# Three of a kernel's four layer multiplications as seven products of quarters, with VectorE alone on the weights' low parts in two of them

## The chip, the cores and the metric

The kernel runs on one core of a Trainium2 chip. The metric is the time of one execution on the device, in microseconds; each kernel is run several times and the median stands for it. TensorE multiplies matrices (PE in the profile, its weight loads are PEld), VectorE (DVE), ScalarE (ACT) and GpSimd (POOL) work element by element, and SyncE (SP) issues the transfers between HBM and the on-chip memory SBUF. TensorE writes its sums to PSUM. The engines run their own lists of instructions in order and wait for each other by semaphores.

## The reference

Attention over 2 batches, 12 heads, 448 positions and 64 dimensions a head, whose scores go through a soft cap, and then two layers that are each a multiplication, an activation and a second multiplication:

```python
scores = cap * np.tanh(scale * np.matmul(q, k.transpose(0, 1, 3, 2)) / cap)
scores = scores - np.max(scores, axis=-1, keepdims=True)
attn = np.exp(scores); attn = attn / (np.sum(attn, axis=-1, keepdims=True) + 1e-09)
x = np.matmul(attn, v)                     # then to 896 rows (tokens) x 768
h = x @ w_in                               # layer 1: 768 x 2048
g = np.where(h > 0.0, h, np.exp(np.minimum(h, 0.0)) - 1.0)
y = g @ w_out                              # 2048 x 768
h2 = y @ w_in2; g2 = np.maximum(0.01 * h2, h2); out = g2 @ w_out2     # layer 2
```

All inputs and the output are float32. (The lines above are the reference's own, drawn together.)

## The kernel before

TensorE multiplies in the format fp32r, which keeps fewer bits than float32. So each operand is split into a high part (rounded to fp32r) and a low part (the rest), and each tile is three matmuls: high by high, high by low, low by high (`product`, L579 to L583). A matmul has 448 columns, the tokens of one batch.

The attention works through 48 slots (24 heads, two halves each) in `STEPS` = 55 steps, each engine with its own list over the steps. In a step TensorE makes eight transposes (`transposes`, L554), four score matmuls for the next slot (`score`, L535) and, every second step, eight value matmuls (`values`, L568). ScalarE makes tanh, two exponentials and a copy; VectorE the maxima (L434), the low part of the probabilities (L441) and small steps; GpSimd splits q, k and v and makes the parts of x (`x_parts`, L289).

The layers are four passes: batch 0 through layer 1 and layer 2, then batch 1. A pass has 32 units, 16 for its first multiplication and 16 for its second; a unit is one load of 128 x 768 weights, whose high part ScalarE makes (L375) and whose low part GpSimd makes (L307, one instruction that subtracts), and 18 matmuls (3.65 us of TensorE). Raw weights have three buffers (`RAW`), the parts four (`RING`), and they are prepared three units ahead (`AHEAD`). Weights of each layer are loaded once for each batch, 128 loads in all. A hidden tile is activated by ScalarE (L383, L385, or L387) and VectorE (L467 or L470) and split by VectorE (L472, L474); an output tile of layer 1 is split by ScalarE and VectorE (L391, L480), one of layer 2 copied by VectorE and stored (L486, L211).

The passes of batch 0 (64 units) are mixed into steps 30 to 54 (`units_at`, L50), so that TensorE has them between the attention's matmuls of batch 1. Fifteen chunks (three matmuls each) of units 0 to 2 come even earlier, in steps 20 to 29 (`EARLY`). The 64 units of batch 1 follow alone. Semaphores set the order otherwise: a unit's matmuls wait for its low part (`w_split`), its PSUM bank waits for VectorE's last read of the tile three before, ScalarE's high part waits for the matmuls of the unit four before.

## Time and profile before

| | us |
|---|---|
| median of 3 runs (lowest to highest) | 631.44 (630.68 to 632.18) |
| the profiled execution's own time | 628.43 |
| its span, from first to last instruction | 626.4 |

The profile shows one execution. Busy time of an engine is the time in which it had an instruction at work. TensorE's matmuls overlap in their records: one lasts 0.36 us, and the next starts 0.20 us after it started; so the distance between starts is what one costs. Below, each row stands as the profile gives it. L12 is line 12 of the kernel before. `PEclk` or the number before the share of DMA is the clock granted to TensorE, as a part of full speed (1.00 is 2.4 GHz, 0.50 is 1.2 GHz).

### The profile page before, as it was taken

The page shows a single profiled execution, that of the slowest core. Times are in us where ns is not written, and L with a number is a line of the kernel's source. Part 1 is how long each engine was busy: PE and PEld are TensorE (multiplying, and loading weights), DVE is VectorE, ACT ScalarE, POOL GpSimd, SP SyncE. Part 2 cuts the span into 40 slices and gives each one's busy share as a digit, 9 for nine tenths or more (in the row PEclk, how much of TensorE's full clock was granted, in tenths as well). Part 3 has the DMA queues.
Part 4 walks back from the last instruction along what each step waited for, and adds up shares of the span by engine and source line. Part 5 has one row for each costly group of instructions (what it writes and reads, how often), then busy time and mean ns, then how long its engine had stood idle before and what let it go on. Part 6 is the DMA issues. An engine that isn't in the chain of part 4 may idle for free.

```text
span 626.4 us, 8464 instructions
## 1 busy us (share of the span) xinstructions
PE 595.8 (95%) x3072; PEld 539.9 (86%) x3072; DVE 280.7 (45%) x537; ACT 302.3 (48%) x526; POOL 380.5 (61%) x335
## 2 busy tenths in 40 slices
PE   5887789799999999999999999999999999999998
PEld 3666678699999999999999999999999999999997
DVE  5886887685752233466652010454400024551000
ACT  5997887676764454544532221445513223332220
POOL 6799987776757656736538464354645354456450
PEclk9998899999999999999999999999999999999999
DMA  5453333645435414323234434233443333334420
GB/s 161 111 165 89 88 90 98 181 134 129 122 103 142 119 53 139 91 78 116 84 93 130 139 117 142 89 101 102 116 136 102 100 100 101 112 115 141 126 95 29
DMA packets 35320, 70.18 MB, mean 112 GB/s; under 512 B 6992, under 2 KB 18896, under 8 KB 35280
## 3 DMA queue, kind: packets, MB, share of 16 engines
q1 hardware_dynamic: 35280, 69.66, 38.2%
q8 instruction: 24, 0.39, 0.3%
q14 instruction: 16, 0.13, 0.1%
HBM read 66.85 MB, written 2.80 MB: 111 GB/s over the span
## 4 chain that ended last, share of the span: by engine, by line
PE 81%; POOL 7%; DMA 5%; ACT 2%; issue 2%; DVE 1%; SPq 0%; POOLq 0%; ACTq 0%
PE mlp_ps L581 16%; PE mlp_ps L583 16%; PE mlp_ps L582 16%; PE o_ps L581 8%; PE o_ps L582 8%; PE o_ps L583 8%; PE probs_t L564 2%; DMA inv_all<-inv_rows 2%; DMA inv_rows<-row_inv 2%; PE o_ps L575 2%; PE o_ps L576 2%; POOL x_raw L295 1%; PE scores L550 1%; PE scores L551 1%; POOL q_stack L268 1%
## 5 line engine op out<-in xcount | busy, mean ns | idle before, releaser
L307 POOL TENSOR_TENSOR w_lo<-w_raw,w_hi 128x768 fp32r<-128x768 f32 x128 | 235.5, 1846 | 188.0 <-ACT w_hi L375 188.0
L375 ACT ACTIVATE w_hi<-w_raw 128x768 fp32r<-128x768 f32 x128 | 106.2, 838 | 85.5 <-PE mlp_ps L583 53.3
L581 PE MATMUL mlp_ps<-x_hi,w_hi 128*128 128x448 f32 x258 | 95.3, 369 | 1.7 <-POOL x_lo L300 1.7
L582 PE MATMUL mlp_ps<-x_lo,w_hi 128*128 128x448 f32 x258 | 94.4, 366 | 0.0
L583 PE MATMUL mlp_ps<-x_hi,w_lo 128*128 128x448 f32 x258 | 94.4, 366 | 0.0
L581 PE MATMUL mlp_ps<-g_hi,w_hi 128*128 128x448 f32 x256 | 93.9, 367 | 0.0
L583 PE MATMUL mlp_ps<-g_hi,w_lo 128*128 128x448 f32 x256 | 93.6, 366 | 0.0
L582 PE MATMUL mlp_ps<-g_lo,w_hi 128*128 128x448 f32 x256 | 93.6, 366 | 0.0
L434 DVE TENSOR_SCALAR_CACHE_REDUCE soft<-soft,neg_abs 112x448 f32<-112x448 f32 x96 | 60.8, 670 | 17.6 <-ACT soft L348 17.4
L358 ACT ACTIVATE soft<-soft,neg_max 112x448 f32<-112x448 f32 x96 | 63.2, 665 | 3.2 <-DVE soft L434 3.0
L441 DVE TENSOR_TENSOR p_lo<-probs_t,p_hi 112x896 fp32r<-112x896 f32 x38 | 41.3, 1087 | 32.5 <-ACT p_hi L367 32.3
L581 PEld LDWEIGHTS mlp_ps<-x_hi,w_hi 128*128 128x128 f32 x258 | 48.5, 188 | 6.2 <-issue 1.9
L348 ACT ACTIVATE soft<-scores 112x896 f32<-112x896 f32 x47 | 43.0, 914 | 19.7 <-PE scores L551 19.7
L583 PEld LDWEIGHTS mlp_ps<-x_hi,w_lo 128*128 128x128 f32 x258 | 48.4, 188 | 4.0
L582 PEld LDWEIGHTS mlp_ps<-x_lo,w_hi 128*128 128x128 f32 x258 | 48.5, 188 | 3.8
L581 PEld LDWEIGHTS mlp_ps<-g_hi,w_hi 128*128 128x128 f32 x256 | 48.1, 188 | 4.0
L583 PEld LDWEIGHTS mlp_ps<-g_hi,w_lo 128*128 128x128 f32 x256 | 48.1, 188 | 3.9
L582 PEld LDWEIGHTS mlp_ps<-g_lo,w_hi 128*128 128x128 f32 x256 | 48.1, 188 | 3.8
L550 PE MATMUL scores<-k_hi,q_stack 128*112 128x448 f32 x94 | 37.4, 397 | 14.2 <-ACT soft L348 8.3
L367 ACT ACTIVATE p_hi<-probs_t 112x896 fp32r<-112x896 f32 x38 | 34.8, 915 | 25.4 <-PE probs_t L564 25.2
L581 PE MATMUL o_ps<-g_hi,w_hi 128*128 128x448 f32 x128 | 47.0, 367 | 0.0
L582 PE MATMUL o_ps<-g_lo,w_hi 128*128 128x448 f32 x128 | 46.8, 365 | 0.0
(78 smaller groups left out, 1029.1 us busy)
## 6 DMA issues: line engine op xcount, KB each, us to landing
w_raw<-w_units SPq DMA_DIRECT2D x128, 384.0 KB, 3.1
q_raw<-qT SPq DMA_DIRECT2D x24, 224.0 KB, 2.8
k_raw<-kT SPq DMA_DIRECT2D x24, 224.0 KB, 2.5
v_raw<-v_rows SPq DMA_DIRECT2D x24, 112.0 KB, 2.8
inv_all<-inv_rows SPq DMA_DIRECT2D x24, 112.0 KB, 3.1
y_t<-y_out SPq DMA_DIRECT2D x12, 224.0 KB, 2.3
inv_rows<-row_inv SPq DMA_DIRECT2D x24, 1.8 KB, 3.0
cap_col<-cap_value SPq DMA_DIRECT2D x1, 0.5 KB, 4.0
```

The costliest lines, as they stand in the source:

```text
L307: pool.tensor_tensor(w_lo[:, u % RING, :], w_raw[:, u % RAW, :], w_hi[:, u % RING, :].bitcast(F32), ALU.subtract).then_inc(w_split, 1)
L348: nc.scalar.activation(soft[0:QT, k % SOFT, :, :], scores_of(k)[0:QT, :, 0:SEQ], ACT.Tanh, scale=scale_reg).then_inc(tanh_done, 1)
L358: nc.scalar.activation(soft[0:QT, b, t, :], soft[0:QT, b, t, :], ACT.Exp, bias=neg_max[:, c, t:t + 1], scale=-1.0, accum_out=row_sum[:, h ...
L367: nc.scalar.activation(p_hi[:, h % 2, :, half * 2 * QT:(half + 1) * 2 * QT].rearrange("p (a b) q -> p a b q", a=2), probs_of(k)[0:QT, :, 0 ...
L375: nc.scalar.activation(w_hi[:, u % RING, :], w_raw[:, u % RAW, :], ACT.Copy).then_inc(w_hi_done, 1)
L434: nc.vector.tensor_scalar(soft[0:QT, b, t, :], soft[0:QT, b, t, :], neg_abs[0:QT, 0:1], BIG, ALU.mult, ALU.min, accum_out=neg_max[:, c, t: ...
L441: nc.vector.tensor_tensor(p_lo[:, h % 2, :, cols].rearrange("p (a b) q -> p a b q", a=2), probs_of(k)[0:QT, :, 0:SEQ].rearrange("p a (b q) ...
L550: nc.tensor.matmul(dst[0:QT, t, 0:SEQ], q_stack[:, b, rows], k_hi[:, b, :], start=True, stop=False)
L564: last = nc.tensor.transpose(probs_of(k)[0:QT, c // 2, col:col + QT], soft[0:QT, k % SOFT, t, c * QT:(c + 1) * QT], ident[:, :])
L581: nc.tensor.matmul(dst, w_hi[:, r, blk], hi, start=start, stop=False)
L582: nc.tensor.matmul(dst, w_hi[:, r, blk], lo, start=False, stop=False)
L583: return nc.tensor.matmul(dst, w_lo[:, r, blk], hi, start=False, stop=stop)
```

## The change

The first multiplication of layer 1 stays as it was, unit by unit. The three others (layer 1's second, layer 2's first, layer 2's second) are each taken as a multiplication of 2 x 2 quarters: the weights are cut in halves both ways, and the activations in the halves of their features and in the two batches. Instead of eight products of quarters there are seven, in the order `ORDER`, of sums and differences of quarters, and their results are added up. So both batches go through a layer together.

In the second products 28 items (7 products of 4 pairs of tiles, 18 matmuls each) take the place of 32 units. Four of the seven products need a sum or difference of weight quarters, which VectorE makes (`weight_sum`), and four need sums or differences of activations. For all items but the first three, VectorE makes the low part of the weights too (`weight_low`, list `LO_ON_DVE`), and of the activations (`g_low`), while ScalarE makes both high parts. GpSimd makes the weights' low parts for the first three items, for layer 1's first multiplication and for the blocks. The blocks are layer 2's first multiplication: for each of 8 inner indices seven half items of 9 matmuls and half a weight unit each. Before them, the y of layer 1's second product is turned into the seven activations of the blocks (`X_GROUPS`): three are quarters of y, four are sums or differences (`x_sum`), and each is split by ScalarE (`x_high`) and VectorE (`x_low`).

Only layer 1's first 16 units are mixed into the attention, as 81 chunks in steps 31 to 54 (`MIXED`) beside the 15 of before. The raw weights have four buffers, loads are 120. GpSimd, ScalarE, VectorE and SyncE have the new order written out in their lists. Sizes: `PQ` is 4, `PRE` is 3, `FULL2` is 28, `GEMM2[l]` is the number of the first item of layer l's second product, `GEMM1` that of the first half item of the blocks.

The diff, cut to its core:

```diff
-RAW = 3
+HALF = UNIT // 2
+HC = KC // 2
+HF = FC // 2
+LAYER_UNITS = 2 * MAT_UNITS
+FIRST_UNITS = BATCH * MAT_UNITS
+RAW = 4
...
-MIXED = 2 * PASS_UNITS
...
+MIXED = {31: (0, 0, 1), 32: (1, 1, 0), 33: (1, 1, 0), **{s: (2, 2, 0) for s in range(34, 48, 2)},
+         **{s: (1, 1, 0) for s in range(35, 48, 2)}, 48: (2, 1, 0), 49: (1, 2, 0), 50: (2, 1, 0), 51: (2, 0, 4),
+         52: (0, 0, 6), 53: (0, 0, 6), 54: (0, 0, 7)}
...
+ORDER = ("p1", "p5", "p6", "p3", "p7", "p2", "p4")
+SUMS = ("p5", "p6", "p3", "p7")
+QUARTERS = {"p1": (0,), "p5": (2, 3), "p6": (0,), "p3": (1,), "p7": (0, 2), "p2": (1,), "p4": (3,)}
...
+LO_ON_DVE = [n for l in range(2) for n in range(GEMM2[l] + PRE, GEMM2[l] + FULL2)]
+LO_ON_POOL = [n for n in range(ITEMS) if n not in LO_ON_DVE]
+SUM_ITEMS = [n for n in range(ITEMS) if item_name(n)[1] in SUMS]
...
+X_GROUPS = ("p3", "p7", "p1", "p5", "p6", "p2", "p4")
...
+        x_source = {"p3": y22, "p7": y22, "p1": y11, "p5": y12, "p6": y11, "p2": y21, "p4": y21}
...
+            def split_w(n):
+                pool.wait_ge(w_hi_done, n + 1)
+                pool.tensor_tensor(w_part(w_lo, n), w_source(n), f32(w_part(w_hi, n)), ALU.subtract).then_inc(w_lo_pool, 1)
...
+            def x_high(p):
+                if p in ("p3", "p1", "p2"):
+                    act.wait_ge({"p3": y22_done, "p1": y11_done, "p2": y21_done}[p], HC)
+                else:
+                    act.wait_ge(x_sum_done, ("p7", "p5", "p6", "p4").index(p) + 1)
+                nc.scalar.activation(x_parts_of[p][0][:, :, :], x_source[p][:, :, :], ACT.Copy).then_inc(xc_hi_done, 1)
...
+            def second(l):
+                for n in range(PRE, FULL2):
+                    if n == 2 * PQ - 1:
+                        keep(l)
+                    w_high(GEMM2[l] + n)
+                    g_high(l, n)
+                    if l == 0 and n == 24:
+                        x_high("p3")
+                    if l == 0 and n == 26:
+                        x_high("p7")
...
+            second(0)
+            w_high(GEMM1)
+            w_high(GEMM1 + 1)
+            x_high("p1")
+            w_high(GEMM1 + 2)
+            w_high(GEMM1 + 3)
+            x_high("p5")
+            w_high(GEMM1 + 4)
+            w_high(GEMM1 + 5)
+            x_high("p6")
+            w_high(GEMM1 + 6)
+            for q in range(GEMM1, GEMM2[1]):
+                i, k = divmod(q - GEMM1, 7)
+                if k == 0 and i:
+                    leak(i - 1, "p4")
+                if k == 1:
+                    block_keep(i)
+                if ORDER[k - 1] in ("p3", "p7", "p2"):
+                    leak(i, ORDER[k - 1])
+                if q + 7 < GEMM2[1]:
+                    w_high(q + 7)
+                if i == 0 and k == 2:
+                    x_high("p2")
+                if i == 0 and k == 4:
+                    x_high("p4")
...
+            def weight_low(n):
+                dve.wait_ge(w_hi_done, n + 1)
+                nc.vector.tensor_tensor(w_part(w_lo, n), w_source(n), f32(w_part(w_hi, n)), ALU.subtract
+                                        ).then_inc(w_lo_dve, 1)
...
+            def second(l):
+                y = [(y12, y22, y11)[i] if l == 0 else y_out[:, HC * i:HC * i + HC, :] for i in range(3)]
+                for n in range(PRE, FULL2):
+                    if n == 4 * PQ - 1:
+                        dve.wait_ge(p1_kept, HC * l + HC)
+                        add_to(l, "p6", kept_u2[l], kept_p1[l], u2_done)
+                        dve.wait_ge(u2_done, HC * l + HC)
+                        add_to(l, "p5", kept_u4[l], kept_u2[l], u4_done)
+                    if n == 5 * PQ - 1:
+                        dve.wait_ge(u4_done, HC * l + HC)
+                        add_to(l, "p3", y[0], kept_u4[l], y12_done)
+                    if n == 6 * PQ - 1:
+                        add_to(l, "p7", kept_u2[l], kept_u2[l], u3_done)
+                        add_to(l, "p7", y[1], kept_u4[l], y22_done)
+                    if n == 7 * PQ - 1:
+                        add_to(l, "p2", y[2], kept_p1[l], y11_done)
+                    if n + 1 < FULL2 and GEMM2[l] + n + 1 in SUM_ITEMS:
+                        weight_sum(GEMM2[l] + n + 1)
+                    if PQ <= n < 2 * PQ and (l or n - PQ >= PRE):
+                        second_sum(l, n - PQ)
+                    if 5 * PQ <= n < 6 * PQ:
+                        fourth_difference(l, n - 5 * PQ)
+                    if GEMM2[l] + n in LO_ON_DVE:
+                        weight_low(GEMM2[l] + n)
+                    g_low(l, n)
+                    if l == 0 and n == 24:
+                        x_low("p3")
+                    if l == 0 and n == 25:
+                        dve.wait_ge(xc_split, X_GROUPS.index("p3") + 1)
+                        x_sum(y22, y22, y12, ALU.subtract)
+                    if l == 0 and n == 26:
+                        x_low("p7")
...
+            def block_add(i, p):
+
+                ps = block_bank(i, p)
+                dve.wait_ge(unit_done, product_no(i, p))
+                if p == "p6":
+                    dve.wait_ge(block_p1_kept, i + 1)
+                    nc.vector.tensor_tensor(block_u2, block_p1, ps, ALU.add).then_inc(block_u2_done, 1)
+                    dve.wait_ge(block_u2_done, i + 1)
+                    nc.vector.tensor_tensor(block_u4, block_u2, block_bank(i, "p5"), ALU.add).then_inc(block_u4_done, 1)
+                if p == "p3":
+                    dve.wait_ge(block_u4_done, i + 1)
+                    nc.vector.tensor_tensor(ps, block_u4, ps, ALU.add).then_inc(h_done, 1)
+                if p == "p7":
+                    nc.vector.tensor_tensor(block_u2, block_u2, ps, ALU.add).then_inc(block_u3_done, 1)
+                    dve.wait_ge(block_u3_done, i + 1)
+                    nc.vector.tensor_tensor(ps, block_u4, ps, ALU.add).then_inc(h_done, 1)
+                if p == "p2":
+                    nc.vector.tensor_tensor(ps, block_p1, ps, ALU.add).then_inc(h_done, 1)
+                if p == "p4":
+                    nc.vector.tensor_tensor(ps, block_u2, ps, ALU.add).then_inc(h_done, 1)
...
+            second(0)
+            for p in SUMS:
+                weight_sum(GEMM1 + ORDER.index(p))
+            x_low("p1")
+            dve.wait_ge(xc_split, X_GROUPS.index("p1") + 1)
+            x_sum(y12, y12, y11, ALU.subtract)
+            x_low("p5")
+            x_sum(y11, y22, y11, ALU.add)
+            x_low("p6")
+            dve.wait_ge(u3_done, HC)
+            add_to(0, "p4", y21, kept_u2[0], y21_done)
+            for q in range(GEMM1, GEMM2[1] + 1):
+                i, k = divmod(q - GEMM1, 7)
+                if k == 0 and i:
+                    block_add(i - 1, "p4")
+                    block_hidden(i - 1, "p2")
+                    first_difference(1, i - 1)
+                    third_difference(1, i - 1)
+                if k == 1 and i:
+                    block_hidden(i - 1, "p4")
+                if k == 3:
+                    block_add(i, "p6")
+                if k == 4:
+                    block_add(i, "p3")
+                if k == 5:
+                    block_add(i, "p7")
+                    block_hidden(i, "p3")
+                if k == 6:
+                    block_add(i, "p2")
+                    block_hidden(i, "p7")
+                if q + 8 < GEMM2[1] and q + 8 in SUM_ITEMS:
+                    weight_sum(q + 8)
+                if i == 0 and k == 2:
+                    x_low("p2")
+                    dve.wait_ge(xc_split, X_GROUPS.index("p2") + 1)
+                    x_sum(y21, y21, y11, ALU.subtract)
+                if i == 0 and k == 4:
+                    x_low("p4")
+                if q in (GEMM2[1] - 4, GEMM2[1] - 2):
+                    g_low(1, (q - GEMM2[1] + 4) // 2)
+            block_hidden(HF - 1, "p4")
+            g_low(1, 2)
+            second(1)
...
+            def blocks(i, k):
+                p, n = ORDER[k], GEMM1 + 7 * i + k
+                bank_free(i, p)
+                pe.wait_ge(*split_done(n))
+                if i == 0:
+                    pe.wait_ge(xc_split, X_GROUPS.index(p) + 1)
+                r, blk = place(n)
+                for c in range(HC):
+                    last = product(block_bank(i, p), r, blk + c, x_parts_of[p][0][:, c, :], x_parts_of[p][1][:, c, :], c == 0,
+                                   c == HC - 1)
                 last.then_inc(unit_done, 1)
...
+            for u in range(MAT_UNITS, FIRST_UNITS):
+                hidden(u, range(KC))
+            second(0)
+            for i in range(HF):
+                for k in range(7):
+                    blocks(i, k)
+            second(1)
```

## Rows read from the trace of the kernel before

**Rows 1.** Page, part 1: busy time, share of the span, instructions of each engine.
```profile
PE 595.8 (95%) x3072; PEld 539.9 (86%) x3072; DVE 280.7 (45%) x537; ACT 302.3 (48%) x526; POOL 380.5 (61%) x335
```
**Rows 2.** Page, part 4: the chain that ended last, by engine.
```profile
PE 81%; POOL 7%; DMA 5%; ACT 2%; issue 2%; DVE 1%; SPq 0%; POOLq 0%; ACTq 0%
```
**Rows 3.** Stretches: length, then busy PE, PEld, DVE, ACT, POOL; clock, DMA, GB/s.
```profile
75.61:105.64 30.03, 27.32 (x166) 23.85 (x165) 24.43 (x55) 24.33 (x50) 25.41 (x36) 1.00 0.37 98
110.00:310.00 200.00, 195.51 (x1030) 178.30 (x1030) 108.53 (x206) 111.44 (x199) 129.62 (x114) 1.00 0.40 114
310.00:620.00 310.00, 310.00 (x1540) 287.21 (x1539) 85.99 (x137) 99.26 (x147) 159.00 (x92) 1.00 0.37 111
```
**Rows 4.** Timeline (start, duration in us): step 30's first matmuls, and the last ones.
```profile
111.46 0.93 PE L564 MATMUL probs_t<-ident,soft 112*112 112x112 f32 x8
...
622.99 0.36 PE L583 MATMUL mlp_ps<-g_hi,w_lo 128*128 128x448 f32 x1
623.39 0.62 DVE L486 COPY y_out<-mlp_ps 128x448 f32<-128x448 f32 x1 [6.67 <-PE mlp_ps L583]
```
**Rows 5.** Timeline of TensorE, batch 1 alone: 56 matmuls apart.
```profile
399.65 0.36 PE L582 MATMUL mlp_ps<-x_lo,w_hi 128*128 128x448 f32 x1
...
411.00 0.37 PE L581 MATMUL mlp_ps<-x_hi,w_hi 128*128 128x448 f32 x1
```
**Rows 6.** Weight loads to landing (us), and the stretch with the most traffic.
```profile
w_raw<-w_units SPq DMA_DIRECT2D x128, 384.0 KB, 3.1
...
36.00:39.00 3.00, 2.85 (x23) 2.39 (x21) 2.93 (x7) 2.95 (x7) 2.83 (x4) 1.00 0.88 288
```
**Rows 7.** Chain of waits in order of time: start and duration of eight transposes.
```profile
130.81 0.77 PE probs_t L564 x8
```
**Rows 8.** Groups by form (busy us, mean ns), ScalarE.
```profile
L375 ACT ACTIVATE w_hi<-w_raw 128x768 fp32r<-128x768 f32 x128 | 106.2, 838 | 85.5 <-PE mlp_ps L583 53.3 <-PE o_ps L583 24.1 <-DMA w_raw<-w_units 8.1
L348 ACT ACTIVATE soft<-scores 112x896 f32<-112x896 f32 x47 | 43.0, 914 | 19.7 <-PE scores L551 19.7
L385 ACT ACTIVATE act_g<-act_g 128x448 f32<-128x448 f32 x32 | 18.5, 578 | 1.0
L383 ACT ACTIVATE act_g<-mlp_ps 128x448 f32<-128x448 f32 x21 | 11.4, 543 | 31.5 <-PE mlp_ps L583 31.5
```
**Rows 9.** Groups by form, GpSimd's subtractions of 768 and of 448 columns.
```profile
L307 POOL TENSOR_TENSOR w_lo<-w_raw,w_hi 128x768 fp32r<-128x768 f32 x128 | 235.5, 1846 | 188.0 <-ACT w_hi L375 188.0
L265 POOL TENSOR_TENSOR k_lo<-k_raw,k_hi 128x448 fp32r<-128x448 f32 x22 | 25.3, 1150 | 0.0
```
**Rows 10.** Group by form, then the timeline: VectorE with one operand in PSUM.
```profile
L441 DVE TENSOR_TENSOR p_lo<-probs_t,p_hi 112x896 fp32r<-112x896 f32 x38 | 41.3, 1087 | 32.5 <-ACT p_hi L367 32.3
...
402.05 0.63 DVE L467 SCALAR_TENSOR_TENSOR mlp_ps<-act_g,mlp_ps 128x448 f32<-128x448 f32 x1 [1.70 <-ACT act_g L385]
402.71 0.62 DVE L472 CAST g_hi<-mlp_ps 128x448 fp32r<-128x448 f32 x1
```
**Rows 11.** Timeline: VectorE's only instructions with two SBUF inputs, and GpSimd.
```profile
3.93 1.31 POOL L268 TENSOR_TENSOR q_stack<-q_raw,q_stack 64x448 fp32r<-64x448 f32 x1
4.29 1.43 DVE L499 TENSOR_TENSOR k_lo<-k_raw,k_hi 128x448 fp32r<-128x448 f32 x1
...
6.82 0.62 DVE L499 TENSOR_TENSOR k_lo<-k_raw,k_hi 128x448 fp32r<-128x448 f32 x1
```
**Rows 12.** Timeline of TensorE around two short gaps, and the stretch behind.
```profile
45.72 0.43 PE L550 MATMUL scores<-k_hi,q_stack 128*112 128x448 f32 x1 [0.72 <-ACT soft L348]
...
47.61 0.54 PE L575 MATMUL o_ps<-p_hi,v_both 112*128 112x448 f32 x1 [0.85 <-DVE x_raw L460]
...
48.32 0.57 PE L575 MATMUL o_ps<-p_hi,v_both 112*128 112x448 f32 x1
48.69 0.57 PE L576 MATMUL o_ps<-p_lo,v_both 112*128 112x448 f32 x1
...
48.00:51.00 3.00, 3.00 (x11) 2.58 (x10) 2.42 (x7) 2.52 (x6) 2.60 (x4) 0.50 0.83 175
```

More of the change, by code:

```diff
@@ L59, in early_chunks, with chunks_at @@
 def early_chunks(u):
     return [c for parts in EARLY.values() for unit, cs in parts if unit == u for c in cs]
-def layer_of(pas):
-    return pas % 2
-def batch_of(pas):
-    return pas // 2
-def dram_unit(u):
-    return layer_of(u // PASS_UNITS) * PASS_UNITS + u % PASS_UNITS
+LATER = [(u, c) for u in range(MAT_UNITS) for c in range(KC) if c not in early_chunks(u)]
+def chunks_at(s):
+    if s in EARLY:
+        return [], [], EARLY[s]
+    done = sum(sum(n) for t, n in MIXED.items() if t < s)
+    places = []
+    for n in MIXED.get(s, (0, 0, 0)):
+        place = {}
+        for u, c in LATER[done:done + n]:
+            place.setdefault(u, []).append(c)
+        places.append(list(place.items()))
+        done += n
+    return places
@@ new lines, in raw_tables @@
+def raw_tables():
+    rows, reads, last = [], [], {}
+    for n in range(ITEMS):
+        stage, p, j = item_name(n)
+        if stage == "first":
+            rows.append(n % MAT_UNITS)
+            reads.append([len(rows) - 1])
+        elif stage == "blocks":
+            if p == "p1":
+                rows += [LAYER_UNITS + j, LAYER_UNITS + j + HF]
+                r0 = len(rows) - 2
+            reads.append({"p5": [r0 + 1], "p7": [r0, r0 + 1], "p4": [r0 + 1]}.get(p, [r0]))
+        else:
+            base = LAYER_UNITS * (stage == "second1") + MAT_UNITS
+            reads.append([])
+            for q in QUARTERS[p]:
+                rows.append(base + q * PQ + j)
+                reads[-1].append(len(rows) - 1)
+        for r in reads[-1]:
+            last[r] = n
+    return rows, reads, last
@@ new lines, in build, with rows @@
+        v_both = sb("v_both", [QT, 2, NQ, P], F32R, attention)
+        soft = sb("soft", [P, SOFT, 2, SEQ], F32, attention)
+        p_hi, p_lo = (sb(n, [QT, 2, NQ, SEQ], F32R, attention) for n in ("p_hi", "p_lo"))
+        x_raw, inv_all = sb("x_raw", [P, 2, SEQ], F32, attention), sb("inv_all", [P, 2, SEQ], F32, attention)
+        def rows(name, n, stack, dt=F32):
+            return sb(name, [P, n, SEQ], dt, stack)
+        attention.close()
+        y12, y11 = rows("y12", HC, later), rows("y11", HC, later)
@@ new lines, in build @@
+        p3_hi, p3_lo, p7_hi, p7_lo = (rows(n, HC, later, F32R) for n in ("p3_hi", "p3_lo", "p7_hi", "p7_lo"))
+        y22, u4_first = rows("y22", HC, later), rows("u4_first", HC, later)
+        t1_first = rows("t1_first", HF + 1, later)
+        p1_first, u2_first = rows("p1_first", HC, later), rows("u2_first", HC, later)
+        rows("spare", 1, later)
+        g_first = [rows(f"g_first{i}", 4, later, F32R) for i in range(RING)]
+        s_sum = sb("s_sum", [P, RING, UNIT], F32, later)
+        later.close()
@@ new lines, in build @@
+        blocks_place.close()
+        last = ctx.enter_context(ExitStack())
+        p1_last = rows("p1_last", HC, last)
+        rows("y11_place", HC, last)
+        y_out = rows("y_out", 4 * HC, last)
+        rows("p6_hi_p1_hi_place", 2 * HC, last)
+        g_last = [rows(f"g_last{i}", 4, last, F32R) for i in range(RING - 1)]
+        rows("t1_place", HF, last)
+        g_last.append(rows("g_last3", 4, last, F32R))
+        u2_last, u4_last = rows("u2_last", HC, last), rows("u4_last", HC, last)
@@ L411, in _ @@
                     exp(s - 1)
-                for us in units_at(s - 1)[1:]:
-                    for u in us:
-                        unit(u)
+                for u in units_ending_at(s - 1):
+                    unit(u)
                 if 2 <= s <= SLOTS + 1:
```

576 lines of the change are left out of this document (378 added, 198 removed).

## The prediction

> **What bounds the kernel now.** I read the page's busy table first, then its chain, then stretches of the span, then the prices of single instructions. TensorE is busy 95% of the span; the other engines lie between 45% and 61% [rows 1]. The chain that ended last is 81% TensorE [rows 2]. By stretch [rows 3]: between 75.61 and 105.64 us the attention leaves TensorE idle for 2.7 of 30.0 us; from 110 to 310 us, where both layers of batch 0 are mixed into the attention of batch 1, it idles 4.5 of 200 us; from 310 to 620 us it never does. So from about 111.5 us the kernel costs what its matmuls cost, and a shorter list of matmuls shortens it, if the other engines keep step. Step 30 begins with eight transposes at 111.46 us, and the last matmul starts at 622.99 us, with its VectorE reader at 623.39 [rows 4]; the reader starts about 0.03 us after the matmul's modelled end, so I take 623.35 as the end of TensorE's work. That is 511.9 us from step 30 on, of which 4.5 idle.
>
> **What is removed.** A 448-column matmul costs 0.2027 us: 56 of them lie between the starts 399.65 and 411.00 [rows 5]. The clock was fully granted there [rows 3]. Before, each of the four multiplications of two batches (layer 1 first and second, layer 2 first and second) costs 32 units x 18 = 576 matmuls. After, the first stays at 576; each of the three others is seven products of quarters: 28 items x 18 = 504, or 56 half items x 9 = 504. So 3 x 72 = 216 matmuls go: 43.8 us. TensorE's work from step 30 is then 511.9 - 4.5 - 43.8 = 463.6 us, and without any idle it would end at 111.5 + 463.6 = 575.1 us. The first 30 steps are unchanged in their work and stand at what they cost. The weight loads fall from 128 to 120 of 384 KB and land in 3.1 us [rows 6]; where an item needs two loads (8 of 28) it is 786 KB in 3.65 us, 215 GB/s, which lies below the 288 GB/s of one stretch [rows 6]. I cost loads at nothing. The cover is a ring of four buffers, two such items deep; without it each such item would wait a landing.
>
> **Idle that comes back in the attention.** Only 81 chunks (243 matmuls) are now mixed into steps 31 to 54, where 64 whole units were. From step 34 a pair of steps has 8 score, 8 value and 18 weight matmuls (34 x 0.2027 = 6.9 us) and 16 transposes (0.77 us for eight [rows 7], 1.5), so 8.4 us. ScalarE was busy 24.3 us in the four pairs from 75.61 to 105.64, which hold no unit's end [rows 3]: 6.1 a pair, and one unit adds 0.54 + 0.58 + 0.84 [rows 8]: 8.0. GpSimd was busy 25.4 there, 6.4 a pair, and a unit's low part adds 1.85 [rows 9]: 8.2. All three are near each other, so the chain of waits between them shows. In the unfilled steps 75.61 to 105.64 the time was 1.10 of TensorE's busy time [rows 3]; 8.4 x 1.10 = 9.3 a pair. Seven such pairs are 65 us, steps 30 to 33 about 15 (they hold 5 chunks), steps 48 to 54 24.2 of matmuls and 2 of gaps: 106 us, against 96.2 us of matmuls (399 x 0.2027 and 160 transposes). Idle: 10 us; bounds 4.5 (the rate of before) and 20 (10.7 a pair).
>
> **Prices on VectorE.** An instruction of 448 columns costs 0.62 and one of 896 costs 1.09 with one operand in PSUM [rows 10]; that is 0.16 + 0.00103 x columns, and 0.66 from start to start [rows 10]. The change leans on another kind: both inputs in SBUF. Only L499 is of that kind, twice: 0.62 when GpSimd was idle, 1.43 when GpSimd's subtraction L268 had started at 3.93 and ran to about 5.2 [rows 11]: it waited that out and then took its 0.62. So the price alone is that of PSUM, and beside GpSimd it adds the rest of GpSimd's instruction. The Trainium skill (SBUF — State Buffer, Who interferes with whom) says the same: such an instruction and a GpSimd one that reads SBUF exclude each other for the whole instruction; had they shared bandwidth, the blocks below would be some 1.7 us an inner index lighter. With gaps: 384 columns 0.60, 768 0.99, 896 1.13, 1344 1.59.
>
> **The two second products.** GpSimd has nothing in them but three low parts each, so VectorE runs alone. An item gives TensorE 3.65 us. VectorE's 25 items (the first three are prepared earlier) hold 25 x (0.99 + 1.13) = 53.0, 16 weight sums 15.8, 8 sums of activations 9.0 and 18 PSUM additions 11.9: 90 us against 25 x 3.65 = 91.2. For layer 1 it is five of the activation sums (three are done before) and three 1344-column instructions: 91. ScalarE has 0.84 + 0.95 an item, half of it. So VectorE is as loaded as TensorE. What saves the pace is order: the common item costs 3.1; the heavy ones (n = 15 and 23, about 7) follow after stretches of light ones, an item's preparation may start when item n-4 is done, 10.9 us ahead, and needs 1.8 of ScalarE and 3.1 of VectorE. I take 0 for the pace, up to 10 a stage if waits break the order.
>
> **From layer 1's second product to layer 2's blocks.** Here VectorE makes five of the blocks' seven activations, each a sum (three PSUM additions of 0.66, or one of 1.59 in SBUF), a ScalarE copy (1.3: 0.54 to 0.91 from 448 to 896 columns [rows 8], extended) and a low part (1.59), one after another, with GpSimd now subtracting half units of 1.01 (1.846 - 384 x 0.00218, the slope of 1.150 to 1.846 [rows 9]) and excluding it. With 0 at the end of the sixth product: VectorE's y11 at 5.7, last item's low part 7.8, four weight sums 11.1, p1's parts at 13.7 (needed 14.6), p5's at 19.3 (needed 16.4: TensorE waits 2.9), p6's at 24.4 (needed 21.0: 3.4), y21 at 26.4, p2's at 30.8 (0.9), p4's at 39.6, because its ScalarE copy is queued behind the leak of p3, which waits for VectorE's addition (needed 32.6: 7.0). Sum 14.2; without the exclusion 10.7. I take 12.5, bounds 8 and 18. A gap this long can cost the clock as well: after idle of 0.72 and 0.85 us close together, the granted clock was 0.50 over 48 to 51 us, 1.2 GHz, and matmuls came 0.37 us apart [rows 12]. Nine matmuls so are 1.5 us more. I add 2, bounds 0 and 4.
>
> **The blocks.** Per inner index TensorE has 63 matmuls, 12.8 us. VectorE has 11 PSUM instructions (7.3), four sums of 384 (2.4) and two of 448 in SBUF (1.3): 11.0, and GpSimd's 7 x 1.01 is 55% of the time, so each of the six SBUF ones meets it with 0.55 and waits 0.5: 1.7. Sum 12.7, against 12.8. The eight banks let VectorE lag about five blocks. I take 2 us over eight indices, bounds 0 and 8. At the start of the last product VectorE still owes 5.3 us of the last index and a low part, then items of 4.2 us: item 7 comes about 1 us late. I take 1, bounds 0 and 4.
>
> **Tail.** From 623.35 to the span's end at 626.4 are 3.05 us (an addition, a DMA). After, the last item is ordered by tile, so again one addition and one DMA follow: 3.05.
>
> Sum: 575.1 + 10 + 12.5 + 2 + 2 + 1 = 602.6; + 3.05 = 605.7 of span; + 2.0 outside the span (628.4 - 626.4) = 607.7 for a profiled execution, 20.7 less than 628.4. The median of the runs before, 631.4, is 1.0048 of the profiled time; so I forecast 610.5 as the median.
>
> **Rivals.** (A) The transition is covered better than my hand schedule says: with VectorE ahead and stalls of 5 us, no lost clock, attention pairs at 8.9: 607.7 - 7.5 - 2 - 3 = 595, median 598. For it: the chain has slack at the start. Against: five activations in series. (B) The pace of VectorE rules in the products: 90 of 91 leaves nothing for the waits between ScalarE and VectorE, and each second product lasts 8 us longer, or the attention pairs take 10.7: 10 to 16 us more, 620 to 626. For it: the loads above; against: 9 us of preparation time an item. (C) Slower: an SBUF-only instruction in the second products costs more than L499's single 0.62. Of the 90 us a stage 78 are of this kind. The gain still to lose is 20.7; over two stages 10.3 each, so it decides from a factor of 1.14 (768 columns at 1.13 instead of 0.99). At the mean of the two L499 rows, 1.03 over 0.62 = 1.64, each stage takes 50 us longer: 607.7 + 100 = 708. Against it: the high row has GpSimd's instruction beside it, and GpSimd is empty there. (D) The gain isn't there because half weight units (384 columns, 9 matmuls) break TensorE's rhythm: at 0.2027 + 10% in the blocks, 504 matmuls, 10 us more: 620. Against: matmuls have no other pitch where a tile and its bank change between them, 56 in a row at 0.2027 cross three such changes [rows 5].
>
> **How the numbers follow.** Forecast 0.57 (602 to 618), A 0.14, B and D 0.20, C 0.08, else 0.01. The range takes A's and most of B's: 597 to 627. A measurement of this kernel can tell about 0.2% from no change. Faster: all but C and a small rest of B: 0.90; same 0.02; slower 0.08.
>
> **What would show it.** Matmuls fall from 3072 to 2856. Step 30 at 111 us as before. The attention's end (last value matmuls) some 106 us after step 30, less the fillers behind. In the second products VectorE at over 90% busy and TensorE without idle; if TensorE idles there in front of w_lo or g_lo, B or C. An SBUF-only 768-column instruction at 0.95 refutes C. After layer 1's second product TensorE waits for the parts of p5, p6 and p4, 13 us in all, the last longest. In the blocks VectorE's two-input SBUF instructions have a mean above their price alone.

## The result

| | before | changed kernel |
|---|---|---|
| median of the runs, us (lowest to highest) | 631.06 (630.47 to 632.18, 4 runs) | 607.13 (605.08 to 608.88, 4 runs) |
| profiled execution, us | 628.43 | 605.08 |
| its span, us | 626.4 | 603.3 |

The ratio is 0.9618, with a 95% interval of 0.9576 to 0.9659: 3.8% faster. Measured again beside the experiments it was 0.9648 (0.9628 to 0.9668). Where I compare an experiment with the changed kernel below, I take the mean of the two, 0.9633, and one thousandth of the ratio is 0.63 us.

The changed kernel's page, busy time of the engines and the slices of the span (against [rows 1]):

```profile
PE 556.1 (92%) x2856; PEld 500.4 (83%) x2856; DVE 469.8 (78%) x712; ACT 357.0 (59%) x607; POOL 285.9 (47%) x301
...
PE   4786799879998999999999999769999999999997
...
DVE  5887778876776413699898999779998868999881
...
PEclk9999999999999999999999999889999999999999
```

TensorE has 216 matmuls fewer, and VectorE went from 281 to 470 us of work, with 90% or more in 12 of the 40 slices. TensorE's slices are at 90% or more from the 14th on, except two (7 and 6), in which the granted clock falls too (8), and the last one. The two are the passage from layer 1's second product to the blocks.

The same kernel by stretches (columns as in [rows 3]); they are the attention from step 30 on, the rest of it with layer 1's first and second products, the passage, the blocks, the start of layer 2's second product and its rest:

```profile
112.87:200.00 87.13, 78.22 (x460) 69.00 (x459) 62.21 (x129) 73.46 (x141) 70.16 (x84) 1.00 0.43 113
...
200.00:380.00 180.00, 180.00 (x890) 166.83 (x889) 135.56 (x148) 92.20 (x129) 56.44 (x34) 1.00 0.38 122
380.00:410.00 30.00, 21.05 (x88) 18.38 (x87) 23.60 (x27) 12.77 (x21) 15.80 (x11) 0.89 0.17 52
410.00:500.00 90.00, 90.00 (x446) 83.40 (x445) 77.47 (x115) 41.20 (x80) 50.06 (x44) 1.00 0.22 67
500.00:530.00 30.00, 28.53 (x139) 25.36 (x138) 27.78 (x32) 16.42 (x22) 0.00 (x0) 1.00 0.47 158
530.00:600.00 70.00, 70.00 (x346) 64.50 (x344) 55.62 (x68) 28.18 (x34) 0.00 (x0) 1.00 0.38 129
```

TensorE idles 8.9 us in the first, 9.0 in the third and 1.5 in the fifth, and nowhere else after step 30. Step 30 begins at 112.87 and the last matmul starts at 599.88 (the timeline of TensorE):

```profile
112.87 0.93 PE L1007 MATMUL probs_t<-ident,soft 112*112 112x112 f32 x8
...
599.88 0.37 PE L1026 MATMUL scores<-g_last,w_lo 128*128 128x448 f32 x1
```

Against [rows 4] step 30 came 1.4 us later. The arithmetic before it is the same in both kernels, but one thing isn't: with four raw buffers, step 8 loads four weight units and not three. The loads as SyncE issues them, in the kernel before and in the changed one, and a wait of TensorE that the kernel before doesn't have:

```profile
35.79 1.38 SPq L202 DMA_DIRECT2D w_raw<-w_units  x3
...
35.89 2.48 SPq L425 DMA_DIRECT2D w_raw<-w_units  x4
...
PE o_ps L1018 <- POOL v_both L490: 5.2, 2, 3.4
```

The next load of v is issued at 44.52 us instead of 42.41, and TensorE waits 3.36 us at 56.85 for its split. No run tests whether the fourth load is the cause, and there is scatter besides: the eleven other traces with this beginning reach step 30 between 113.0 and 115.5 us, all later than the one trace of the kernel before. The last matmul starts 23.1 us earlier.

Now the passage. The first fence is TensorE, the second VectorE, the third ScalarE:

```profile
384.54 0.37 PE L1026 MATMUL o_ps<-p_hi,w_lo 128*128 128x448 f32 x1
388.05 0.44 PE L1024 MATMUL mlp_ps<-p_hi,w_hi 128*128 128x448 f32 x1 [3.15 <-DVE p_lo L821]
...
390.96 0.57 PE L1024 MATMUL scores<-p_hi,w_hi 128*128 128x448 f32 x1
391.33 0.57 PE L1025 MATMUL scores<-p_lo,w_hi 128*128 128x448 f32 x1
...
396.77 0.36 PE L1026 MATMUL probs_t<-p_hi,w_lo 128*128 128x448 f32 x1
402.94 0.71 PE L1024 MATMUL mlp_ps<-p_hi,w_hi 128*128 128x448 f32 x1 [5.81 <-DVE p_lo L821]
```

```profile
378.17 1.56 DVE L825 TENSOR_TENSOR y<-y 128x1344 f32<-128x1344 f32 x1
381.12 1.56 DVE L821 TENSOR_TENSOR p_lo<-y,p_hi 128x1344 fp32r<-128x1344 f32 x1 [1.39 <-ACT p_hi L611]
382.59 2.37 DVE L825 TENSOR_TENSOR y<-y 128x1344 f32<-128x1344 f32 x1
386.35 1.56 DVE L821 TENSOR_TENSOR p_lo<-y,p_hi 128x1344 fp32r<-128x1344 f32 x1 [1.39 <-ACT p_hi L611]
...
394.55 2.26 DVE L825 TENSOR_TENSOR u_first<-u_first,y 128x1344 f32<-128x1344 f32 x1
...
401.24 1.56 DVE L821 TENSOR_TENSOR p_lo<-u_first,p_hi 128x1344 fp32r<-128x1344 f32 x1 [2.23 <-ACT p_hi L611]
```

```profile
399.04 0.54 ACT L628 ACTIVATE act_g<-scores 128x448 f32<-128x448 f32 x1 [5.99 <-DVE scores L871]
399.48 0.51 ACT L580 ACTIVATE w_hi<-s_sum 128x384 fp32r<-128x384 f32 x1
399.89 1.31 ACT L611 ACTIVATE p_hi<-u_first 128x1344 fp32r<-128x1344 f32 x1
```

Each part is a sum, ScalarE's copy and a low part, in series: VectorE stands idle for 1.39 us behind each of the first two sums while ScalarE copies. The last one is worst, and as the step on the passage said: the sum for p4 is ready at 396.8, but its copy starts only at 399.89, behind the leak of p3 (L628) for which ScalarE waits 5.99 us. Behind both gaps matmuls come 0.37 us apart, as in [rows 12]: 9 of them after the first gap (from 388.73 us on, the fourth matmul), 7 after the second. From the start behind each gap until the pitch is 0.20 us again, the matmuls took 3.0 us more than at that pitch.

### The profile page after: what moved, and what is told of

The parts are those of the page before. It is cut to its first block and busy times, and to the rows that moved or that the text cites. A ratio compares the mean times of both kernels' runs of the same rounds, so it can differ in the third digit from the quotient of the medians.

```text
span 603.3 us, 8512 instructions
## 1 busy us (share of the span) xinstructions
PE 556.1 (92%) x2856; PEld 500.4 (83%) x2856; DVE 469.8 (78%) x712; ACT 357.0 (59%) x607; POOL 285.9 (47%) x301
## 5 line engine op out<-in xcount | busy, mean ns | idle before, releaser
L516 POOL TENSOR_TENSOR w_lo<-w_raw,w_hi 128x768 fp32r<-128x768 f32 (+1 forms) x62 | 101.8, 1644 | 151.6 <-ACT w_hi L580 150.9
L580 ACT ACTIVATE w_hi<-s_sum 128x768 fp32r<-128x768 f32 (+1 forms) x64 | 43.9, 686 | 75.4 <-DVE s_sum L806 51.9
L580 ACT ACTIVATE w_hi<-w_raw 128x768 fp32r<-128x768 f32 (+1 forms) x80 | 59.1, 741 | 33.0 <-PE o_ps L1026 15.7
L516 POOL TENSOR_TENSOR w_lo<-s_sum,w_hi 128x384 fp32r<-128x384 f32 x32 | 38.4, 1219 | 32.5 <-ACT w_hi L580 32.5
L1024 PE MATMUL mlp_ps<-x_hi,w_hi 128*128 128x448 f32 x132 | 49.4, 374 | 0.0
L1007 PE MATMUL probs_t<-ident,soft 112*112 112x112 f32 x304 | 37.3, 267 | 11.9 <-DVE p_lo L711 11.0
L1025 PE MATMUL mlp_ps<-x_lo,w_hi 128*128 128x448 f32 x132 | 48.2, 365 | 0.0
L1026 PE MATMUL mlp_ps<-x_hi,w_lo 128*128 128x448 f32 x132 | 48.2, 365 | 0.0
L1018 PE MATMUL o_ps<-p_hi,v_both 112*128 112x448 f32 x96 | 36.3, 378 | 10.0 <-POOL v_both L490 5.2
L1019 PE MATMUL o_ps<-p_lo,v_both 112*128 112x448 f32 x96 | 35.8, 373 | 0.0
```

The costliest lines, as they stand in the source:

```text
L516: pool.tensor_tensor(w_part(w_lo, n), w_source(n), f32(w_part(w_hi, n)), ALU.subtract).then_inc(w_lo_pool, 1)
L580: nc.scalar.activation(w_part(w_hi, n), w_source(n), ACT.Copy).then_inc(w_hi_done, 1)
L1007: last = nc.tensor.transpose(probs_of(k)[0:QT, c // 2, col:col + QT], soft[0:QT, k % SOFT, t, c * QT:(c + 1) * QT], ident[:, :])
L1018: nc.tensor.matmul(o_bank, v_both[:, b, c, :], p_hi[:, b, c, :], start=(c == 0), stop=False)
L1024: nc.tensor.matmul(dst, w_hi[:, r, blk], hi, start=start, stop=False)
L1025: nc.tensor.matmul(dst, w_hi[:, r, blk], lo, start=False, stop=False)
```

## The experiments

**Is the passage a series of parts?** In e1 the blocks use p3's parts for all seven products, and those of p1, p5, p6, p2 and p4 are not made (on VectorE's or ScalarE's list), so layer 2 works on other data.

```diff
-                    last = product(block_bank(i, p), r, blk + c, x_parts_of[p][0][:, c, :], x_parts_of[p][1][:, c, :], c == 0,
+                    last = product(block_bank(i, p), r, blk + c, p3_hi[:, c, :], p3_lo[:, c, :], c == 0,
...
-            x_sum(y12, y12, y11, ALU.subtract)
-            x_low("p5")
-            x_sum(y11, y22, y11, ALU.add)
-            x_low("p6")
```

> The changed kernel again, as the measure for its neighbours. Its first ratio to the kernel before was 0.962. Both theories of the next runs expect 0.962 within 0.004 here; the runs of it so far fell at 605.1 to 605.6 and at 608.7 to 608.9, so I also want to see whether this spread of 3 us comes back.

> The seven blocks all take the activation parts of p3, and the sums, copies and low parts for p1, p5, p6, p2 and p4 are left out, so layer 2 works on other data. Theory S (the parts are made in series, and TensorE waits for them): the two gaps in front of p6 and p4 (9.4 us by the starts of the matmuls) and the half-clock matmuls behind them (3.1 us) go, TensorE has under 1 us of idle from 380 to 410 us, the span falls by 12 us, the ratio to 0.943. Rival W (the blocks' weights are late: sums on VectorE, copies on ScalarE, low parts on GpSimd all start at that place too): the gaps stay for the greater part, the span falls by 0 to 4 us.

c0: 0.9648, and all its runs lay at 608.7 to 609.9, beside the upper two of the first four; the lower value of 605 didn't come back. I use the mean. e1: 0.9431 (0.9412 to 0.9451), 12.7 us less than the changed kernel, and its stretch of the passage is full:

```profile
380.00:410.00 30.00, 30.00 (x149) 27.80 (x149) 22.56 (x34) 12.96 (x27) 17.79 (x17) 1.00 0.18 54
```

Theory S holds and W falls: the weights were ready.

**The same work in another order.** e2 leaves nothing out:

```diff
             x_sum(y12, y12, y11, ALU.subtract)
-            x_low("p5")
             x_sum(y11, y22, y11, ALU.add)
+            x_low("p5")
             x_low("p6")
             dve.wait_ge(u3_done, HC)
             add_to(0, "p4", y21, kept_u2[0], y21_done)
+            dve.wait_ge(xc_split, X_GROUPS.index("p6") + 1)
+            dve.wait_ge(y21_done, HC)
+            x_sum(y11, y21, y11, ALU.subtract)
+            x_low("p2")
+            x_low("p4")
```

ScalarE's copies move in the same way (p6 right behind p5; p2 and p4 before the loop of the blocks), and p4's source is now y11.

> All the work is kept, only the order changes: VectorE makes the sum for p6 before p5's low part, puts p4's sum into y11 right after y21 and makes the low parts of p2 and p4 before the loop; ScalarE copies p5 and p6, and p2 and p4, one behind the other, ahead of the leaks. Theory S with the durations of the profile: p6's parts 3.5 us earlier, p4's about 10 us earlier, both before TensorE asks for them; the span falls by 9 to 12 us, the ratio to 0.943 to 0.948. Rival X (what sets the time there is the exclusion between GpSimd's low parts and VectorE's sums, not the order): VectorE has the same sum of work and blocks in the same place, the span falls by at most 5 us.

0.944 (0.9415 to 0.9465), median 595.73 us, 12.2 us less than the changed kernel. Theory S again. e2's VectorE at the same place, two sums and then two low parts without an idle gap, and its stretch:

```profile
378.29 3.03 DVE L823 TENSOR_TENSOR y<-y 128x1344 f32<-128x1344 f32 x2
381.25 3.03 DVE L819 TENSOR_TENSOR p_lo<-y,p_hi 128x1344 fp32r<-128x1344 f32 x2
...
380.00:410.00 30.00, 30.00 (x148) 27.27 (x147) 29.29 (x35) 15.47 (x26) 17.71 (x14) 1.00 0.18 54
```

VectorE is busy 29.3 of the 30 us instead of 23.6: the cost of the passage was order, not load, and the exclusion (its instructions still meet GpSimd's: 1344-column ones of 2.37 instead of 1.55 follow in e2 as well) had only to be covered.

**Who makes the low parts in the second products?** e4 and e3 give them back to GpSimd, all or every second one:

```diff
-LO_ON_DVE = [n for l in range(2) for n in range(GEMM2[l] + PRE, GEMM2[l] + FULL2)]
+LO_ON_DVE = []
```

(e3 has the old line with `if n % 2 == 0` at its end.)

> GpSimd instead of VectorE makes the low parts of the weights in both second products. Theory X (instructions of VectorE with two SBUF inputs and GpSimd's subtraction exclude each other): an item with a weight sum then costs the two together 1.85 + 0.87 + 1.00 = 3.72 us, one with an activation sum too 4.7, against TensorE's 3.65, so TensorE waits in items 4 to 15: 3 to 6 us a stage, the span is 5 to 12 us longer than that of the changed kernel, and the means of w_lo on GpSimd and g_lo on VectorE lie clearly above 1.85 and 1.09. Rival R (VectorE's relief of 22 us a stage is what counts): no idle, same time as the changed kernel within 1 us or faster by the 1.6 us that TensorE waits at the start of layer 2's second product.

> GpSimd makes the weights' low parts of every second item of the second products, VectorE the others. All on GpSimd cost 17 us more than the changed kernel. Theory X (mutual exclusion; GpSimd's subtraction takes 1.85 where VectorE needs 0.87): each item moved adds at most 1 us of the pair's common time, and an average item stays below 3.65 (about 2.8 + 0.5 = 3.3), only the stretch with activation sums goes over it: the span 1 to 6 us longer than the changed kernel. Rival R (sharing relieves VectorE, as its instructions in between can run on): the same or up to 2 us shorter.

e4: 0.991 (0.988 to 0.994), 17.5 us more than the changed kernel. e3: 0.9707 (0.9669 to 0.9745), 4.7 us more, inside theory X's 1 to 6, though its interval only just clears that of the changed kernel (up to 0.9668). So most of this kernel's gain over the one before hangs on VectorE doing this alone. e4's timeline, VectorE and then GpSimd:

```profile
308.06 1.08 DVE L766 TENSOR_TENSOR g_first<-b,g_first 128x896 fp32r<-128x896 f32 x1
309.06 0.95 DVE L806 TENSOR_TENSOR s_sum<-s_sum,w_raw 128x768 f32<-128x768 f32 x1
309.93 2.74 DVE L766 TENSOR_TENSOR g_first<-b,g_first 128x896 fp32r<-128x896 f32 x1
312.60 2.60 DVE L806 TENSOR_TENSOR s_sum<-s_sum,w_raw 128x768 f32<-128x768 f32 x1
```

```profile
309.09 5.28 POOL L516 TENSOR_TENSOR w_lo<-s_sum,w_hi 128x768 fp32r<-128x768 f32 x2 [1.77 <-ACT w_hi L580]
```

The same instruction takes VectorE 1.08 alone and 2.74 beside GpSimd's, the sum 0.95 and 2.60. GpSimd's took 2.6 each in place of 1.85 [rows 9]. They alternate: from 309.93 to 312.60 us, 2.67 us, lie one instruction of VectorE (1.00 at its pitch alone) and 1.67 us for GpSimd, which needs 1.85. At most 0.2 us run side by side. Theory X holds, its size was too small (5 to 12 us expected): TensorE meets the shortage where the six PSUM additions of n = 15 come on top. It waits there in both stages (of TensorE's waits):

```profile
PE mlp_ps L1024 <- DVE u_last L817: 4.9, 1, 4.9
...
PE mlp_ps L1024 <- DVE u_first L817: 4.3, 1, 4.3
```

Behind the two waits 8 and 16 matmuls come 0.37 us apart, for which X's estimate had no term.

**How much room has VectorE there?** e5 adds work to its list: `extra` is one addition of 384 columns into a place that nobody reads (it waits for the `extra` of the item before, which is long done).

```diff
+                    extra(l)
                     g_low(l, n)
```

> One more addition of 384 columns (two SBUF inputs, a place nobody reads) in each of the 25 items on VectorE, in both second products: 25 x 0.47 = 11.8 us more a stage. Theory P (my forecast: VectorE has 90 of TensorE's 91.2 us a stage, gaps of 0.04 us between instructions): the stage becomes 10 us longer each time, the span 20 us. Rival Q (what the timeline shows: independent instructions start 0.53, 0.87 and 1.00 us apart for 448, 768 and 896 columns, less than their durations, so that a stage is 78 to 80 us of work): 90 to 92 against 91.2, the span grows by 0 to 5 us.

0.9837 (0.9797 to 0.9878): 12.9 us more for 23.5 us of added work. Between the theories. P's price is wrong: instructions that don't wait for each other start closer than they last (the sum at 309.06 and the next at 309.93: 0.87 for a duration of 0.95). Q's conclusion doesn't follow either. Layer 1's second product from 280 to 380 us, first in the changed kernel (c0's trace), then in e5, and e5's waits of TensorE in the two stages:

```profile
280.00:380.00 100.00, 100.00 (x495) 92.71 (x495) 92.21 (x101) 51.04 (x63) 9.16 (x6) 1.00 0.44 140
...
280.00:380.00 100.00, 97.89 (x483) 90.40 (x483) 97.54 (x123) 48.70 (x60) 5.32 (x3) 1.00 0.44 139
```

```profile
PE mlp_ps L1032 <- DVE u_first L817: 2.1, 1, 2.1
...
PE mlp_ps L1032 <- DVE u_last L817: 3.2, 1, 3.2
PE scores L1032 <- DVE g_last L766: 2.6, 4, 1.6
```

In the changed kernel VectorE stood idle for 7.8 of these 100 us (some of the rest was already work for the passage), so 11.8 us more don't fit; from 500 to 600 us it idled 16.6, in its first trace. TensorE meets the shortage in bursts (u_first, u_last), and a third of the cost lies outside the two stages: in the passage, which VectorE reached later, TensorE idled 10.5 instead of 9.4 us by starts in e5, and 33 matmuls instead of 17 (c0) came 0.37 us apart.

**The exclusion in the blocks.** e8 puts their low parts on VectorE as well, from the eighth half item on.

```diff
+LO_ON_DVE = sorted(LO_ON_DVE + list(range(GEMM1 + 7, GEMM2[1])))
...
+                if q + 7 < GEMM2[1]:
+                    weight_low(q + 7)
```

> In the blocks of the changed kernel VectorE makes the weights' low parts too (49 of 56), so GpSimd stands still there but for the first seven. Theory X (exclusion): the means of VectorE's instructions with two SBUF inputs in the steady blocks fall to their prices alone (384 columns 0.55 instead of 0.84 to 1.17, 448 columns at L749 0.62 instead of 1.34), so the 3.3 us an index that are added (7 x 0.47) cost VectorE only 1.5 to 2 us net; VectorE stands at 11 to 12.5 of 12.8 us, and the span stays within 0 to 5 us of the changed kernel, most of it at the transition, which is VectorE's. Rival Y (those long means have another reason, such as both inputs in one buffer): they stay, VectorE needs 14 us an index, and the stage grows by 8 to 10 us.

0.9759 (0.9731 to 0.9787), 7.9 us more: outside what X expected. Its mechanism is right all the same. Groups from 415 to 485 us, first the changed kernel, then e8:

```profile
L806 DVE TENSOR_TENSOR s_sum<-w_raw 128x384 f32<-128x384 f32 x10 | 8.6, 856 | 0.0
L749 DVE TENSOR_TENSOR b<-b 128x448 f32<-128x448 f32 x6 | 7.4, 1226 | 0.2
L806 DVE TENSOR_TENSOR s_sum<-w_raw,s_sum 128x384 f32<-128x384 f32 x5 | 5.8, 1162 | 0.7
```

```profile
L807 DVE TENSOR_TENSOR s_sum<-w_raw 128x384 f32<-128x384 f32 x9 | 5.0, 552 | 0.0
L807 DVE TENSOR_TENSOR s_sum<-w_raw,s_sum 128x384 f32<-128x384 f32 x4 | 2.2, 554 | 0.0
L811 DVE TENSOR_TENSOR w_lo<-s_sum,w_hi 128x384 fp32r<-128x384 f32 x18 | 10.0, 555 | 5.1 <-ACT w_hi L581 5.1
L811 DVE TENSOR_TENSOR w_lo<-w_raw,w_hi 128x384 fp32r<-128x384 f32 x14 | 7.8, 557 | 5.0 <-ACT w_hi L581 5.0
```

With GpSimd silent, 856 and 1162 ns become 552 and 554. VectorE's busy time fell, to 59.3 from 62.3 of 70 us, though it does more. What I left out is a new wait: the low part stands in VectorE's own list right behind ScalarE's copy, and VectorE waits 10.1 us for it in these 70 us. It falls behind, and TensorE waits at the end of the blocks and at the start of layer 2's second product (4.4 us from 490 to 520, against 1.5 in the changed kernel), with 12 matmuls 0.37 us apart behind that.

**The start of layer 2's second product.** e6 makes item 3's low part before all else.

```diff
             block_hidden(HF - 1, "p4")
+            weight_low(GEMM2[1] + PRE)
             g_low(1, 2)
```

> Low part of item 3's weights first: before g's low part of item 2 and before the sum of item 4 at the start of layer 2's second product, ahead of the sum at the start of layer 1's; all else as in the changed kernel. Theory F (VectorE's gap of 2.15 us at 505.9 us is a weight load that can be issued only when item 3's raw weights are free, because the first two-load item finds the ring of four full): the low part ends 1.9 us earlier, the gap and TensorE's waits of 1.4 us and the smaller ones behind it (2.6 us in all) shrink to under 1, the span falls by about 2 us. Rival G (VectorE's debt from the last block alone makes the start late): the gap's time goes to other instructions and TensorE waits as before, 0 us.

0.9621 (0.9593 to 0.9649), no measurable gain. In the changed kernel, the end of the low part, the issue of five loads, and VectorE's gap:

```profile
503.90 0.95 DVE L810 TENSOR_TENSOR w_lo<-w_raw,w_hi 128x768 fp32r<-128x768 f32 x1
504.77 1.08 DVE L766 TENSOR_TENSOR g_last<-b,g_last 128x896 fp32r<-128x896 f32 x1
508.00 0.96 DVE L806 TENSOR_TENSOR s_sum<-w_raw 128x768 f32<-128x768 f32 x1 [2.15 <-issue]
```

```profile
504.88 4.92 SPq L425 DMA_DIRECT2D w_raw<-w_units  x5
```

The load is issued at 504.88, at the end of the low part, and the sum starts 3.12 us later, one landing. F's mechanism is right: in e6 the gap is 0.18. (Layer 1's second product has a gap of 2.03 us at the same place, in front of the sum at 288.87; TensorE doesn't feel that one.) But the low part pushed item 2's g_lo back, and TensorE waited 1.13 us in front of item 2 instead of 1.19 in front of item 4. e9 takes the place between and has e2's order too; e10 is e9 with a fuller mix (four and three chunks in steps 32 and 33, in place of two and two, three fewer in step 54). The first cut is in both, the second in e10 alone:

```diff
+                    if n == PRE:
+                        weight_low(GEMM2[l] + n)
                     if n + 1 < FULL2 and GEMM2[l] + n + 1 in SUM_ITEMS:
...
-MIXED = {31: (0, 0, 1), 32: (1, 1, 0), 33: (1, 1, 0), **{s: (2, 2, 0) for s in range(34, 48, 2)},
+MIXED = {31: (0, 0, 1), 32: (2, 2, 0), 33: (1, 2, 0), **{s: (2, 2, 0) for s in range(34, 48, 2)},
```

> e2's order, and at the start of each second product item 3's low part between g's low part of item 2 and the sum of item 4 (not ahead of g's, as in e6, where TensorE then waited 1.3 us for g's). Theory F (the load of item 5's weights is issued when item 3's raw weights are free): VectorE's gap of 2.15 us shrinks by 0.87, TensorE's wait in front of item 4 falls from 1.35 to about 0.5, the span is 1 us shorter than e2's, the ratio 0.942 to 0.943. Rival G: no difference to e2's 0.944.

> e9, with 5 chunks in step 32 and 33 (in place of 2 and 2, so 7 in all) and three fewer in step 54. Theory M (TensorE idles between 113 and 130 us, 4 us of it, because too little is mixed in there): three chunks are 1.8 us of work moved into idle time, the span is 1.5 to 2 us shorter than e9's. Rival B (ScalarE sets the pace there: three tiles end within two steps and it has 2 us of work for each, it is busy 9.9 of 10 us from 120 to 130): the steps become longer by what is added, no gain, 0 to 1 us either way.

e9: 0.9433 (0.9404 to 0.9461), VectorE's gap is 1.27 us, TensorE's wait in front of item 4 0.17 and its idle from 490 to 520 0.44. So F's mechanism again; that it is worth 1 us isn't shown, since against e2 the difference is inside the intervals. e10: 0.9394 (0.9368 to 0.942), median 592.41 us, the fastest kernel of this study, with nothing left out. Its intervals overlap e9's, but its trace shows the step: from step 30 to the first matmul of layer 1's second product are 164.3 us instead of 165.8, and TensorE's idle in the attention's stretch is 7.2 instead of 8.9 us:

```profile
112.87:200.00 87.13, 79.91 (x468) 70.43 (x467) 62.78 (x133) 74.70 (x144) 70.53 (x83) 1.00 0.43 114
```

So theory M, with 1.5 us of the 1.5 to 2 that it promised, and B's longer steps didn't come. ScalarE was busy 15.5 of 17.1 us there in e9 (from 112.87 to 130), and the three chunks fitted all the same.

**What sets the pace of the attention?** e7 puts the probabilities' parts ahead of the hidden tile, on ScalarE and VectorE.

```diff
-                for u in units_ending_at(s - 1):
-                    unit(u)
                 if 2 <= s <= SLOTS + 1:
                     p_high(s - 2)
+                for u in units_ending_at(s - 1):
+                    unit(u)
```

(Shown is ScalarE's list; in VectorE's, `p_low(s - 2)` moves ahead of `hidden(u)` in the same way.)

> One swap in the mixed steps: ScalarE and VectorE first make the two parts of the probabilities (p_hi, p_lo) and only then work on the finished hidden tile and the next weights. Theory A (the idle of 8.9 us between 112.87 and 200 us comes from p_lo being late behind the hidden tile's 2 us on ScalarE; the transposes wait for it 15 times, 10.9 us in the whole kernel): idle there falls by 3 to 5 us and the span with it, the waits of the transposes for p_lo halve. Rival B (the pace of a pair of steps is set by ScalarE's or GpSimd's load, 8.0 and 8.2 us a pair): the wait moves to another place and the span stays within 1 us.

0.9634 (0.9612 to 0.9656): no difference to the mean of 0.9633. The transposes' wait for p_lo is 9.9 us (11 times) instead of 11.0 (15 times), and the idle of the stretch 9.4 instead of 8.9. Theory A falls. That B's loads are the cause isn't shown by this; it stays open which of the chained waits is late first.

## Why the prediction was right, point by point

The forecast was a median of 610.5 and came out at 607.1, the profiled execution at 605.1 for a forecast of 607.7. Its terms, from step 30 to the end; measured is the distance between starts less what the matmuls cost, unless it says otherwise:

| term, us | forecast | measured |
|---|---|---|
| step 30 begins | 111.5 | 112.9 |
| matmuls removed | 216, 43.8 | 216; no change of pitch: 446 matmuls in 90 us of the blocks |
| matmuls and transposes left | 463.6 | 461.1 (see below) |
| idle in the attention | 10 | 11.2 (8.9 by the profile's idle, up to 200 us) |
| passage, idle | 12.5 | 9.4 |
| passage, half clock | 2 | 3.0 |
| blocks | 2 | 0 |
| start of layer 2's second product | 1 | 1.8 |
| pace of the second products | 0 | 0 |
| small delays of about 0.1 us at waits; modelled end of the last matmul | 0 | 0.8 |
| end of TensorE's work (sum) | 602.6 | 600.2 |
| tail | 3.05 | 3.1 |

**The sum** was nearer than its terms. The beginning of step 30, the attention's idle, the half clock, the start of layer 2's second product and the small delays came out 5.2 us dearer together, the passage and the blocks 5.1 cheaper; that they cancel is luck. What is left is a slip of the sum itself. The 463.6 were taken from the span of before less its 4.5 us of idle, but the profile counts idle only from a matmul's modelled end, 0.16 us after the next could have started, so some idle stays in. Counted, there are 2199 matmuls of 448 columns after step 30 (2199 x 0.2027 = 445.7) and 160 transposes (15.4): 461.1. The forecast took the attention's idle against such a count (96.2 us), so the 2.5 us of idle hidden in the 463.6 came on top.

**The first 30 steps** were taken as unchanged in their work, at no cost; the fourth raw buffer was overlooked there. The 1.4 us stand against a scatter of 2.6 us between traces.

**The passage** was right in place, order and kind. p6 was forecast to wait 3.4 us and waited 3.3, p4 7.0 and 6.0. The mis-sized terms are p5 (2.9; 0.15) and p2 (0.9; nothing). The hand schedule let VectorE come too late there; the 0.04 us that it added behind every instruction, where the trace has them start before the last one ends, go that way, but no run shows that they are the whole of it.

**VectorE's prices.** One SBUF instruction of 768 columns takes 0.956 us, as the line through 448 and 896 columns said, so rival C is refuted. Added gaps were the wrong part: instructions that don't depend on each other start 0.53, 0.87 and 1.00 us apart (448, 768, 896 columns; the latter two in e4's fence, the first from 388.36 to 388.89 us), and the 0.66 in [rows 10] belongs to a chain where each waits for the one before. So a common item costs 2.74, not 3.1, and the listed work of a stage some 80 us, not 90 (an estimate from these distances). The sign of over 90% busy came true in layer 1 (92% from 280 to 380 us, with the first work for the passage in it) and not in layer 2 (83% from 500 to 600). Rival B had its ground in the load; e5 and e4 show what happens when the room is used up. Rival D falls with the pitch of the blocks.

**The blocks.** The exclusion was forecast at 1.7 us an index and is real: the groups above (0.30 more in ten sums, 0.61 in five, 0.60 in six differences, over 5.5 indices) give 1.8. That it cost nothing agrees with the shorter pitch: from 410 to 500 us VectorE was busy 11.0 us an index instead of 12.7. The waits of 10.1 us that e8 added there did cost.

**Loads at nothing** was a step that failed, by little: the cover (a ring of four) is missing at the first two-load items, where item 3's raw weights hold the ring up. That is the 2.15 us gap on VectorE. In e9, where it is 1.27, TensorE's wait in front of item 4 falls from 1.0 (e2) to 0.17 us, so most of the 0.8 us more at the start goes with it.

**Rival A** (the passage covered, median 598) wasn't this kernel's case, but e2 reached it (595.7) by an order that my hand schedule could have found: the forecast named the copy of p4 behind the leak as the cause.

## What to carry to other kernels

When fewer matmuls are bought with more element-wise work, the price shows first where a stage hands over to the next: list there, for each part, sum, copy and low part in the order of the engines' lists, and issue every instruction that another engine waits for before one that waits itself. Leave two engines that exclude each other apart: giving work back to an idle GpSimd cost 17 us here. A load average below 100% isn't room; count the bursts. And a sum of forecast terms needs one measure of idle throughout: starts, or the profile's idle, not both.

## What the runs showed of the hardware

- VectorE instructions without a dependence overlap by about 0.09 us: 0.95 long, 0.87 apart at 768 columns. With a dependence 0.62 long, 0.66 apart (448 columns).
- Exclusion with GpSimd costs both: 2.74 for 1.08 on VectorE, 2.6 for 1.85 on GpSimd. Instructions of VectorE with one operand in PSUM stayed at 0.61 to 0.63 beside GpSimd.
- How many matmuls came at 1.2 GHz behind a gap didn't go by its length: 9 after 3.15 us of idle and 7 after 5.81 in the changed kernel, 16 after 4.31 and none after 3.14 in e4, 14 after 3.14 in e7.
